# Gathering an expert's tokens as quarter rows and turning them on VectorE, in a fused attention, mixture-of-experts and MLP kernel

## Reference

```
attention:  xread = softmax(x state^T / 8) state      sread = softmax(state x^T / 8) x
            rows  = concat(xread, sread) -> N = 8*(512+32) = 4352 tokens of DM = 512
experts:    logits = cosine(rows, expert_emb) / tau;  e = argmax;  gate = softmax(logits)[e]
            rows[t] = gate * (relu(rows[t] @ w1[e]) @ w2[e])     E = 8, w1 512x1024, w2 1024x512
MLP:        h = rows @ w_in (512x2048);  g = max(h,0) + alpha*min(h,0);  out = g @ w_out (2048x512)
```

## Time and profile before

| | before |
|---|---|
| device time, three runs | 1466.27, 1466.37, 1466.83 us |
| median | 1466.37 us |
| span of the profiled execution | 1464.0 us |
| TensorE busy | 1380.0 us (94%) |
| VectorE busy | 641.1 us (44%) |
| ScalarE busy | 398.3 us (27%) |
| GpSimd busy | 191.8 us (13%) |
| mean granted TensorE clock | 0.975 |

### The profile page before, as it was taken

How to read it: one execution, slowest core, us unless ns; L and a number is a source line. 1 busy time by engine, 2 the same in 40 slices (tenths; PEclk the granted TensorE clock), 3 DMA queues, 4 the chain that set the end, 5 groups by cost and what they waited for, 6 DMA issues and landing times.

```text
span 1464.0 us, 18906 instructions
## 1 busy us (share of the span) xinstructions
PE 1380.0 (94%) x6852; PEld 1132.3 (77%) x6853; DVE 641.1 (44%) x919; ACT 398.3 (27%) x634; POOL 191.8 (13%) x235
## 2 busy tenths in 40 slices
PE   4998469999979999996999999999999999999998
PEld 4877358888868888885887888888888888888887
DVE  3677643222545435345544334443443434434343
ACT  5887312111333313224212121121211212112121
POOL 4564122111212222121000000000000000000000
PEclk9999679999989999998999999999999999999999
DMA  7785143111425224143101010010100101001000
GB/s 268 267 263 174 64 144 129 43 43 36 158 100 201 101 100 158 43 158 136 44 0 58 0 57 0 0 57 0 57 0 0 57 0 57 0 0 58 1 29 15
DMA packets 56795, 112.58 MB, mean 77 GB/s; under 512 B 5184, under 2 KB 19520, under 8 KB 56128
## 3 DMA queue, kind: packets, MB, share of 16 engines
q1 hardware_dynamic: 50656, 92.31, 18.5%
q0 software_dynamic: 6112, 19.93, 3.9%
HBM read 84.17 MB, written 27.53 MB: 76 GB/s over the span
## 4 chain that ended last, share of the span: by engine, by line
PE 90%; DVE 3%; DMA 2%; ACT 2%; issue 1%; SPq 0%; ACTq 0%; POOL 0%; DVEq 0%; POOLq 0%
PE ps L314 9%; PE ps L316 9%; PE ps L315 9%; PE ps_o L316 8%; PE ps_o L314 8%; PE ps_o L315 8%; PE ps_h L314 5%; PE ps_h L316 5%; PE ps_h L315 5%; PE ps_y L314 5%; PE ps_y L316 5%; PE ps_y L315 5%; PE ps_hT L1178 2%; PE ps_sr L1087 1%; PE ps_xT L1172 1%
## 5 line engine op out<-in xcount | busy, mean ns | idle before, releaser
L741 ACT ACTIVATE gT_hi<-act_g 128x512 fp32r<-128x512 f32 (+1 forms) x144 | 87.7, 609 | 571.5 <-DVE act_g L1009 571.5
L1006 DVE TENSOR_SCALAR neg<-ps,alpha 128x512 f32<-128x512 f32 (+1 forms) x144 | 103.8, 721 | 299.3 <-PE ps L316 299.3
L314 PE MATMUL ps<-yT_hi,w_hi 128*128 128x512 f32 (+1 forms) x576 | 221.2, 384 | 1.4 <-DVE yT_lo L996 1.4
L316 PE MATMUL ps<-yT_hi,w_lo 128*128 128x512 f32 (+1 forms) x576 | 221.1, 384 | 0.0
L315 PE MATMUL ps<-yT_lo,w_hi 128*128 128x512 f32 (+1 forms) x576 | 221.0, 384 | 0.0
L314 PE MATMUL ps_o<-w_hi,gT_hi 128*128 128x512 f32 x544 | 213.3, 392 | 0.0
L316 PE MATMUL ps_o<-w_hi,gT_lo 128*128 128x512 f32 x544 | 212.4, 390 | 0.0
L315 PE MATMUL ps_o<-w_lo,gT_hi 128*128 128x512 f32 x544 | 211.8, 389 | 0.0
L1012 DVE TENSOR_TENSOR gT_lo<-act_g,gT_hi 128x512 fp32r<-128x512 f32 (+1 forms) x144 | 95.4, 663 | 97.3 <-ACT gT_hi L741 97.3
L314 PE MATMUL ps_h<-w_hi,xgT_hi 128*128 128x512 f32 x296 | 122.8, 415 | 9.2 <-DVE w_lo L770 7.7
L314 PEld LDWEIGHTS ps<-yT_hi,w_hi 128*128 128x128 f32 x576 | 108.7, 189 | 25.1 <-DVE yT_lo L996 1.8
(11 more groups left out here) (179 smaller groups left out, 1749.2 us busy)
## 6 DMA issues: line engine op xcount, KB each, us to landing
stage<-in_moe_w SPq DMA_DIRECT2D x32, 1024.0 KB, 5.1
xs_all<-in_xT SPq DMA_DIRECT2D x8, 1024.0 KB, 6.4
xN_all<-in_xN SPq DMA_DIRECT2D x8, 1024.0 KB, 6.1
rows_x<-xrow SPq DMA_DIRECT2D x32, 256.0 KB, 2.5
yg<-rows_y SPq DMA_DIRECT2D x32, 256.0 KB, 2.7
out_rows<-orow SPq DMA_DIRECT2D x32, 256.0 KB, 2.0
stage<-in_moe_w_in SPq DMA_DIRECT2D x4, 1024.0 KB, 4.8
stage<-in_moe_w_out SPq DMA_DIRECT2D x4, 1024.0 KB, 5.2
```

Of the source, the lines that this page charges most:

```text
L314: pe.matmul(out, s_hi, m_hi, start=start, stop=False)
L316: return pe.matmul(out, s_lo, m_hi, start=False, stop=stop)
L741: act.activation(gT_hi[:, c % 2, f, 0:w], act_g[:, 0:w], ACT.Copy).then_inc(g_hi_ready, 1)
L1006: dve.tensor_scalar(neg[:, 0:w], ps_1[f][:, 0:w], 0.0, alpha[:, ft:ft + 1], ALU.min, ALU.mult)\
```

## The change

- `rows_x` is also viewed as quarter rows of 128 elements (`quarters_x`). `gather` fetches a slot by four indirect DMAs of 128 quarter rows each. Partition 32i+b gets, in `xg[:, j, :]`, quarter i of the token in place 32j+b. The indices for it are spread over the partitions by four small matmuls (`spread`, `src`, `ps_src`) in the index stage.
- With this layout a transpose in 32x32 blocks gives the wanted `xgT`. VectorE makes it in one instruction (`turn_x`), from SBUF to SBUF. The four TensorE transposes of a slot and the tile `ps_xT` are gone. The rows of `w1` are re-ordered on the host to fit.
- `turn_x(s + 1)` is the first thing in VectorE's slot `s`, ahead of the copy of `ps_h[0]`. `x_hi` waits for the slot's second hidden half as well, since it is now free to run earlier. `xg_read`, for which the next gather waits, is raised by `turn_x`.
- On TensorE `transpose_h(s, 0)` stands after 5 matmuls of the second hidden half (6 before), and `transpose_h(s, 1)` after 5 result matmuls (3 before).
- Some small tiles of the index stage are laid over others, and a few small constants are added.

The diff, cut to its core:

```diff
@@ tiles
+        quarters_x = rows_x.rearrange("n (i d) -> (n i) d", i=QB)      # QB = 4, Q = 32
-        gather_idx = sb("gather_idx", [P, SPLUS], U32)
+        gather_idx = sb("gather_idx", [P, SPLUS, QB], U32)
-        xg = sb("xg", [P, DM], c=sc)
+        xg = sb("xg", [P, QB, P], c=sc)
+        xgT = sb("xgT", [P, KD, P], c=sc)
-        ps_xT = pb("ps_xT", [P, KD, P], c=pc)
@@ GpSimd
             def gather(s):
 
-                pool.tensor_copy(gather_now[:], gather_idx[:, bass.ds(s, 1)]).then_inc(gather_set, 1)
+                pool.tensor_copy(gather_now[:], gather_idx[:, bass.ds(s, 1), :].rearrange("p a j -> p (a j)"))\
+                    .then_inc(gather_set, 1)
                 wait_apart(pool, gather_set, s + 1)
-                pool.indirect_dma_start(xg[:], None, rows_x[:, :],
-                                        bass.IndirectOffsetOnAxis(gather_now[:], 0)).then_inc(gathered, 16)
+                for j in range(QB):
+                    pool.indirect_dma_start(xg[:, j, :], None, quarters_x,
+                                            bass.IndirectOffsetOnAxis(gather_now[:, j:j + 1], 0)).then_inc(gathered, 16)
@@ ScalarE
             def x_hi(n):
                 act.wait_ge(xg_read, n)
-                act.activation(xgT_hi[:], ps_xT[:], ACT.Copy).then_inc(xT_hi_ready, 1)
+                if not (isinstance(n, int) and n == 1):
+                    act.wait_ge(h_ready, 2 * n - 2)
+                act.activation(xgT_hi[:], xgT[:], ACT.Copy).then_inc(xT_hi_ready, 1)
@@ VectorE, index stage
             choose(0, XT, 0)
+            ts = [P, QB, QB, Q]
+            step(dve.tensor_tensor(spread, iota_p[:, 0:Q].unsqueeze(1).unsqueeze(1).to_broadcast(ts),
+                                   row_of[:].unsqueeze(2).unsqueeze(2).to_broadcast(ts), ALU.is_equal))
...
             dve.wait_ge(index_summed, 1)
+            dve.tensor_copy(src[:, 1, :], ps_idx[:, 1, :]).then_inc(src_ready, 1)
+            step(dve.tensor_scalar(spare, ps_idx[:, 0, :], 0.0, float(NT + 1), ALU.is_equal, ALU.mult))
+            dve.tensor_tensor(src[:, 0, :], ps_idx[:, 0, :], spare, ALU.add).then_inc(src_ready, 1)
...
-            dve.tensor_scalar(gather_idx[:], idx_f[:], float(N), None, ALU.min)
+            dve.wait_ge(src_spread, 1)
+            step(dve.tensor_scalar(src_h, ps_src[:, :, 0, :], float(QB * P), quad[:, 0:1], ALU.mult, ALU.add))
+            dve.scalar_tensor_tensor(out=gather_idx[:].rearrange("p s j -> p j s"), in0=ps_src[:, :, 1, :],
+                                     scalar=float(QB), in1=src_h, op0=ALU.mult, op1=ALU.add)
             dve.tensor_copy(scatter_idx[:], idx_f[:]).then_inc(index_ready, 1)
@@ VectorE, slots
+            def turn_x(s):
+
+                if not isinstance(s, int):
+                    dve.wait_ge(xT_lo_ready, s)
+                dve.wait_ge(gathered, 16 * QB * s + 16 * QB)
+                dve.transpose(xgT[:].rearrange("p q (j b) -> p j q b", j=QB),
+                              xg[:].rearrange("p j (q a) -> p j q a", q=KD)).then_inc(xg_read, 1)
 
             def slot(s):
+                turn_x(s + 1)
                 for c in range(2):
                     dve.wait_ge(h_ready, 2 * s + c + 1)
@@ TensorE
+            pe.wait_ge(src_ready, 2)
+            for j in range(QB):
+                mm = pe.matmul(ps_src[:, j, :, :], spread[:, j, :, :].rearrange("p i b -> p (i b)"), src, start=True, stop=True)
+            mm.then_inc(src_spread, 1)
...
-            def transpose_x(s):
-                pe.wait_ge(gathered, 16 * s + 16)
-                for k in range(KD):
-                    mm = pe.transpose(ps_xT[:, k, :], xg[:, k * P:(k + 1) * P], ident[:])
-                mm.then_inc(xg_read, 1)
...
             def slot(s, buf):
+                n, early = 3 * KD, 5
                 pe.wait_ge(xT_lo_ready, s + 1)
-                hidden(0, range(KD), buf).then_inc(h_ready, 1)
-                hidden(1, range(0, 2), buf)
+                hidden(0, 0, n, buf).then_inc(h_ready, 1)
+                hidden(1, 0, early, buf)
                 transpose_h(s, 0)
-                hidden(1, range(2, KD), buf).then_inc(h_ready, 1)
-                transpose_x(s + 1)
+                hidden(1, early, n, buf).then_inc(h_ready, 1)
                 pe.wait_ge(yrow_ready, s + 1)
                 pe.wait_ge(hT_lo_ready, 2 * s + 1)
-                result(0, range(0, 1), buf)
+                result(0, 0, early, buf)
                 transpose_h(s, 1)
-                result(0, range(1, KF // 2), buf)
+                result(0, early, n, buf)
                 pe.wait_ge(hT_lo_ready, 2 * s + 2)
-                result(1, range(KF // 2), buf).then_inc(y_ready, 1)
+                result(1, 0, n, buf).then_inc(y_ready, 1)
```

More of the change, by code:

```diff
@@ L52 @@
 PB = 9
+Q = 32
+QB = P // Q
 TINY = 1e-30
@@ L75, in build @@
         w_lo = [sb("w_lo0", [P, CH * CW], F32R)]
-        gather_idx = sb("gather_idx", [P, SPLUS], U32)
+        gather_idx = sb("gather_idx", [P, SPLUS, QB], U32)
         scatter_idx = sb("scatter_idx", [P, SPLUS], U32)
-        gather_now = sb("gather_now", [P, 1], U32)
+        gather_now = sb("gather_now", [P, QB], U32)
         scatter_now = sb("scatter_now", [P, 1], U32)
@@ L169, in build @@
         idx_f = sb("idx_f", [P, SPLUS], c=ab)
-        iota_i = sb("iota_i", [P, P], I32, c=ab)
+        iota_i = stail[:, 0, 0:P].bitcast(I32)
         iota_p = sb("iota_p", [P, P], c=ab)
-        dump_i = sb("dump_i", [P, SPLUS], I32, c=ab)
+        dump_i = stail[:, 0, P:P + SPLUS].bitcast(I32)
         dump = sb("dump", [P, SPLUS], c=ab)
@@ L177, in build @@
         lane = sb("lane", [P, 1], c=ab)
+        quad_i = sb("quad_i", [P, 1], I32, c=ab)
+        quad = sb("quad", [P, 1], c=ab)
+        row_i = sb("row_i", [P, QB], I32, c=ab)
+        row_of = sb("row_of", [P, QB], c=ab)
+        spread = a1[0][:, 0, :].bitcast(BF16).rearrange("p (j i b) -> p j i b", j=QB, i=QB)
+        src_h = a1[0][:, 1, 0:QB * SPLUS].rearrange("p (j s) -> p j s", j=QB)
+        src = a1[0][:, 2, 0:SPLUS].bitcast(BF16).rearrange("p (a s) -> p a s", a=2)
+        spare = a1[0][:, 3, 0:SPLUS]
         back_i = sb("back_i", [P, E], I32, c=ab)
@@ L223, in build @@
         ps_idx = ps_x[:, 0, 0:2 * SPLUS].rearrange("p (a s) -> p a s", a=2)
+        ps_src = ps_x[:, 1, 0:QB * 2 * SPLUS].rearrange("p (j a s) -> p j a s", j=QB, a=2)
         pa.close()
@@ L270, in build @@
         gathered, xg_read = sem("gathered"), sem("xg_read")
+        src_ready, src_spread = sem("src_ready"), sem("src_spread")
         xT_hi_ready, xT_lo_ready = sem("xT_hi_ready"), sem("xT_lo_ready")
@@ L416, in _ @@
             wait_apart(sp, xT_lo_ready, total + 1)
-            wait_apart(sp, gathered, 16 * total + 32)
+            wait_apart(sp, gathered, 16 * QB * total + 32 * QB)
             wait_apart(sp, scattered, 16 * total)
@@ L460, in _ @@
             pool.memset(zeros[:], 0.0).then_inc(const_ready, 1)
-            pool.iota(iota_i[:], pattern=[[1, P]], base=0, channel_multiplier=0).then_inc(const_ready, 1)
-            pool.iota(dump_i[:], pattern=[[P, SPLUS]], base=N + P, channel_multiplier=1).then_inc(const_ready, 1)
+            pool.iota(iota_i, pattern=[[1, P]], base=0, channel_multiplier=0).then_inc(const_ready, 1)
+            pool.iota(dump_i, pattern=[[P, SPLUS]], base=N + P, channel_multiplier=1).then_inc(const_ready, 1)
             pool.iota(tile_i[:], pattern=[[1, NT]], base=1, channel_multiplier=0).then_inc(const_ready, 1)
@@ L465, in _ @@
             pool.iota(back_i[:], pattern=[[-1, E]], base=E, channel_multiplier=0).then_inc(const_ready, 1)
-            pool.wait_ge(const_ready, 10)
+            pool.iota(row_i[:], pattern=[[-Q, QB]], base=0, channel_multiplier=1).then_inc(const_ready, 1)
+            pool.wait_ge(const_ready, 11)
             pool.affine_select(out=ident[:], in_=ident[:], compare_op=ALU.not_equal, fill=1.0, base=0,
@@ L470, in _ @@
                                pattern=[[1, P]], channel_multiplier=-1).then_inc(const_ready, 1)
-            pool.wait_ge(const_ready, 12)
+            pool.wait_ge(const_ready, 13)
             pool.dma_start(rows_x[N:N + 1, :], zrow).then_inc(zero_stored, 16)
@@ L827, in turn @@
                     dve.tensor_copy(srow[:], ps_sr[0:NS, :]).then_inc(sr_copied, 1)
-            dve.wait_ge(const_ready, 12)
-            dve.tensor_copy(iota_p[:], iota_i[:]).then_inc(const_cast, 1)
-            dve.tensor_copy(dump[:], dump_i[:]).then_inc(const_cast, 1)
+            dve.wait_ge(const_ready, 13)
+            dve.tensor_copy(iota_p[:], iota_i).then_inc(const_cast, 1)
+            dve.tensor_copy(dump[:], dump_i).then_inc(const_cast, 1)
             dve.tensor_copy(tile_no[:], tile_i[:]).then_inc(const_cast, 1)
@@ L835, in _ @@
             dve.tensor_copy(lower[:], lower_f[:]).then_inc(const_cast, 1)
+            dve.tensor_copy(row_of[:], row_i[:]).then_inc(const_cast, 1)
+            dve.tensor_scalar(quad_i[:], lane_i[:], 5, None, ALU.arith_shift_right).then_inc(const_cast, 1)
```

(27 more changed lines are left out.)

3 lines of the change are left out of this document (1 added, 2 removed).

## The result

The changed kernel takes 1502.07 us (median of 4 runs, 1499.19 to 1503.49), the kernel before in the same comparison 1466.60 us (4 runs, 1466.27 to 1467.40). The ratio is 1.024, with an interval of 1.0225 to 1.0254: 2.4% slower. The forecast was 1469, with 1461 to 1503 as its range, so it had the side right and the size wrong: +2.7 us against +35.5. The profiled execution took 1499.19 us, the shortest of the four.

What follows compares the result with a forecast made beforehand. TensorE's own queue was taken to bound the expert stage. Terms -15.2 + 11.0 + 2.6 + 3.3 + 1.0 = +2.7 us on the profiled 1464.0, with 2.4 around it, gave 1469 us, range 1461 to 1503.

Steps and rivals of the forecast that it cites:

- GpSimd becomes the bound: Rival: gathers at 1.75 us each, the fourth also misses the first turning slot; +52, 1518 us, chance 0.14.
- What is removed, -15.2: TensorE: one transpose group of 0.433 us gone per slot, counted in 35 slots, -15.2 us.
- The transpose and its place, +11.0: VectorE: 0.69 us transpose behind `w_lo` delays the `ps_h[0]` copy in 12 passages, 0.92 each, +11.0 us.
- Hand-overs, +2.6: Each slot's two hidden halves: 2.07 us of TensorE cover against 2.22 needed; 0.035 x 2 x 37, +2.6 us (0 to 7).
- The start, +3.3 and +1.0: Start-up: longer index chain and three more gathers bring x later, +3.3 us; `gather(1)` following only then, +1.0.
- GpSimd's four gathers, 0: GpSimd: gathers 1.0 us apart; in the second turning slot the fourth slips ahead of `w_lo` by 0.2 us; no wait.
- fourth gather is shut out: Rival: at 1.1 us or more the fourth gather meets `w_lo`; six passages, +7 to +20, 1476 to 1489 us, chance 0.25.
- Faster: Rival: block transpose at 0.35 us and free hand-overs, passages 0.58 each; -4.9, 1461.5 us, chance 0.19.

Runs made afterwards that it cites:

- The last experiment: Changed kernel with gathers ahead of the scatter's landing wait, transpose behind the `ps_h[0]` copy, and result matmuls needing only `hidT_hi` first: 1454.71 us, ratio 0.9923.
- first experiment: Changed kernel with GpSimd's queue alone altered: the next four gathers directly behind the scatter, ahead of the wait for its landing; 1470.61 us, ratio 1.0035.

## Why the prediction was wrong in size, point by point

The range of 1461 to 1503 held, but by luck. It reached so high only for the sake of "GpSimd becomes the bound" (1518), which did not happen. The rival that did happen was put at 1476 to 1489 us, 13 below the measured 1502.07.

**What is removed, -15.2.** Right. The last experiment reaches 12.07 us per plain slot, the very length that the price of 0.433 us for a transpose group gives. The slot that the price was read from stands for even experts only; in odd ones it is 12.28 us, and the last experiment's 11.85 gives the same 0.43.

**The transpose and its place, +11.0.** The mechanism and the time were right: 0.71 us against 0.69, the copy at 3.86 to 3.91 into the slot against 3.87. Its cost came out smaller, 12.87 - 12.22 = 0.65 us for 0.92, and 0.81 in odd experts. With the long slots out of the way (first experiment) that is 8.8 us for twelve. Part of a wait ahead of the copy takes the place of the hand-over waits behind it.

**Hand-overs, +2.6.** Mis-sized. A plain slot is 12.22 us against 12.07, so they cost 0.15 and not 0.07, and 0.21 in odd experts. That is some 6 us for 37 slots; the range named was 0 to 7.

**The start, +3.3 and +1.0.** The sum was right, its parts were not. The first hidden matmul came 0.7 later and slot 0 took 3.7 more, 4.4 in all for 4.3. The index chain was shorter than priced (the gather's indices were copied at 186.94 for 186.56), and x was used 1.7 us behind the last written gather and not 2.4 or more. The wait fell on the gather for slot 1, which can begin only when the first transpose has read `xg`: TensorE waits 3.41 us in slot 0, and the granted clock is 0.73 from 210 to 214 us, behind this wait. The +1.0 stood for the wait alone.

**GpSimd's four gathers, 0.** This is the step that failed. It took the spacing as 1.0 us, from a copy that follows an indirect DMA after 0.02. Two indirect DMAs are 0.95 + 0.30, some 1.26, apart. That put the fourth at 12.2 to 13.0 into the second turning slot and not at 11.7, behind the start of `w_lo` at 11.7. The forecast named this margin, 0.2 us, and what lay behind it, but gave it 0.25 of the chance. A copy's row was no measure for a second DMA's. It also left out that `x_lo` reads SBUF now and can hold the second gather by up to 0.5 us; that was not needed for the miss, since the fourth comes behind `w_lo` at 12.2 without it.

**The rival "fourth gather is shut out".** This is what happened, and its place, its condition (a spacing of 1.1 or more) and its symptom (a record of 2 to 5 us) were right to within a tenth. Its price, +7 to +20 over the forecast, was not; the six slots cost 31.4 us. Three things came out otherwise. The hold was the shorter of the two that it had: the gather is let in between the two chunks (a record of 1.9 to 2.6 us instead of 0.95), for which it had 2.1 us a slot. The landing was longer, 4.35 us behind the end of the record and not 2.4. And five of six waits were followed by a stretch at 1.2 GHz, 1.2 to 2.8 us more a slot beside the one without (17.1 to 18.7 against 15.9). That the clock might fall was named, but not priced. That it is the reading of the indices which is held, as the forecast says, no run shows.

The Trainium skill, SBUF — State Buffer, "SBUF: two separate sides", has the shared port as an exclusive lock. The runs agree that `w_lo` with its two SBUF inputs shuts an indirect DMA out (records of 1.91 and 2.49 us) and a copy from PSUM does not (0.95). They don't agree that the lock lasts for the whole of whichever began first: the gather begun at 392.42, 0.05 ahead of `w_lo`, ran its 0.95 us, and the two chunks took their 4.50 as ever.

**GpSimd as the bound.** Did not happen: at 1.26 us a gather TensorE waits for nothing of GpSimd's in plain slots.

**Faster.** Its conditions were a transpose of 0.35 us and free hand-overs. The transpose takes 0.71, and the hand-overs are not free.

## What to carry to other kernels

One indirect DMA split into four is free only where the issuing queue has room for them. Find the slot with the least room, and lay the records out at the spacing of two indirect DMAs, measured and not borrowed from another instruction. Move waits for landings behind the issues that don't need them. A held issue and a loaded DMA queue may each cost little alone and much together, so price the pair. On an engine that another engine waits for, put the work with slack behind the work without, and let the first matmuls be those whose operands come first.

## What the runs showed of the hardware that was not expected

- Two indirect DMAs of 128 rows follow on GpSimd's queue after a gap of 0.30 to 0.32 us (117 times in the changed kernel), each record 0.95 to 1.0 us where nothing holds it; a copy follows one after 0.00 to 0.02.
- An indirect DMA begun just behind a VectorE `tensor_tensor` with two SBUF inputs ends some 0.85 us after it, with a record of 1.31 to 1.46 us beside `x_lo` and of 1.9 to 2.6 beside a `w_lo` chunk. Begun 0.01 to 0.05 us ahead of it, it takes 0.95.
- A float32 transpose of 128x512 in 32x32 blocks from SBUF to SBUF takes VectorE 0.70 to 0.71 us, as long as a copy from PSUM (0.69).
- The last quarter of a gather of 256 KB was used 1.5 to 1.7 us after it was written in most plain slots (DMA share 0.11 to 0.15 in three of them), and 4.3 to 4.6 us after in the long slots, where a weight load had just begun (DMA share 0.84 in one); with the weight loads cut it was 1.8 to 2.0.
- Of the waits of TensorE in the six long slots, that of 3.42 us was followed by no fall of the granted clock, and those of 3.43, 3.44, 3.66, 3.69 and 3.88 us by stretches at 1.2 GHz. Their length alone does not decide between them; what does was not tried.
